# Top-k attention, routed experts and a Fourier mixer on one core: sign and mask of each even tile formed in two parts

## The chip, the cores and the metric

The kernel runs on one core of a Trainium2 chip. The metric is the device time of one execution in microseconds (us); lower is better. The program is written engine by engine: TensorE (PE in the profile, its weight loads PEld), VectorE (DVE), ScalarE (ACT), GpSimd (POOL) and SyncE (SP) each have their own list of instructions, and only semaphores order one list against another.

## The reference, cut to what matters

Three stages follow each other. Only the first is touched by the change.

```python
# attention: batch 4, heads 8, sequence 576, head_dim 64, top_k 32
scores = scale * np.matmul(q, k.transpose(0, 1, 3, 2))
kth = np.partition(scores, -top_k, axis=-1)[..., -top_k:-top_k + 1]
mask = scores >= kth
scores = np.where(mask, scores, -1000000000.0)
attn = softmax(scores)                     # exp, divided by (sum + 1e-9)
out = np.matmul(attn, v)
# then: each token of 2304 is routed to one of 8 experts (512 -> 1024 -> 512, relu), top-1 with a sequential "keep" gate
# then: real part of a 2-D FFT added, layer norm, a 512 -> 2048 -> 512 relu network, added
```

## The kernel before

**Tiles.** The 32 heads are taken in 16 pairs; a pair's 1152 query rows are nine tiles of 128 rows, which makes `NTILE` = 144 tiles of 128 query rows by 576 key columns. Tiles are worked two at a time ("a pair of tiles", t even and t + 1).

**The way of one pair of tiles.** PE forms the scores in two halves of 288 columns (`scores(k, 0)`, `scores(k, 1)`, L467) into two PSUM banks that both halves share, and ACT copies each half into `s_sb` (`evict_scores`, L657), the first halves before the second halves are computed. DVE forms the larger and the smaller of the two halves (`upper`, L797), GpSimd helps with sums (L743, `sums`) and differences (L753, `lowers`), and DVE finds the 32nd largest value with a chain of MAX8 and MATCH_REPLACE8 (`top_op`, L820 and L822), ended by two scans (L826). ACT forms the exponentials `e_sb` (L648), from the 32nd value a bias (L630, L633), and then `sign` (L637): `Sign(score - kth)` over all 576 columns, +1 where the score is kept, -1 where not. GpSimd multiplies `e_sb` by it (L777), so entries that are not kept become negative. PE transposes the tile in five pieces (`turn`, four of 128 columns into bank `ps_t`, L487, and the last 64 columns into a part of `ps_o`, L493), ACT copies them out with Relu, which sets the negative ones to zero (`turned`, L664 and L666), PE multiplies by the values (`values`, L524), and ACT copies the result out (`result`, L676 and L677).

**The order of the work.** Each engine's loop runs `body(t)` for t from -4 to 147, in the order written. PE, at an even t: scores of the first halves of tiles t+4 and t+5; values of tile t-1; some matmuls of other work (from `units_at`, the first experts' blocks, L186, L201 and L213, for t of 84 and more; before that `keep_clock`, filler matmuls that nobody reads, L502); `turn(t)`; scores of the second halves. At an odd t: filler or other work, `turn(t)`, other work, `values(t-1)`. ACT, at an even t: sign of t and t+1, copies of the first halves of the scores, result of t-1, `turned(t)`, copies of the second halves, two exponentials; at an odd t: `turned(t)`, `result(t-1)`. GpSimd, at an even t: two L753, the mask of t; at an odd t: the mask of t+1 of the pair and then two L743. Gathers and scatters of the experts' tokens (L730, L269) stand ahead of the mask in some of these bodies.

**Semaphores around the change.** `s_sign` counts signs, `s_mask` counts masked tiles. `s_mask` releases `turn(k)` on PE (one wait ahead of all five transposes) and, six tiles later, ACT's copy into the same `s_sb` buffer. For the last two tiles DVE forms the mask (L963) instead of ACT and GpSimd.

```python
pe.wait_ge(s_mask, k + 1)                                        # turn(k)
act.activation(s_sb[k % NS][:, :], s_sb[k % NS][:, :], ACT.Sign, ...).then_inc(s_sign, 1)
pool.wait_ge(s_sign, t + 1)
pool.tensor_tensor(e_sb[t % NE][:, :], e_sb[t % NE][:, :], s_sb[t % NS][:, :], ALU.mult).then_inc(s_mask, 1)
```

Of the kernel before, what the change touches and what calls it, by code (L numbers as in the profile page):

```python
# [12 lines left out]
ALU = mybir.AluOpType  # L13
ACT = mybir.ActivationFunctionType
# [3 lines left out]
B, H, S, D = 4, 8, 576, 64  # L18
# [4 lines left out]
P = 128  # L23
# [256 lines left out]
def attention(nc, env, q_h, k_h, v_h, vt_h):  # L280
# [9 lines left out]
    NS, NW, NE, NT_ = 6, 4, 3, 3  # L290
    HALF_TOP = TOPK // 2
    STEPS = 22
    CLOCK = ((6, 3), (9, 8), (5, 3))
    AHEAD = {MIDDLE + 4: 14, MIDDLE + 6: 4, MIDDLE + 8: 4, MIDDLE + 10: 4}
    SCALE = 1.0 / math.sqrt(D)
# [2 lines left out]
    with ExitStack() as ctx:  # L298
# [6 lines left out]
        def sem(name):  # L305
            return ctx.enter_context(nc.semaphore(name))
# [6 lines left out]
        s_sb = [sb(f"s_sb{n}", [P, S]) for n in range(NS)]  # L313
# [5 lines left out]
        nmax, under, ulp = [kept[:, :, 2 * HALF_TOP + 2 + 2 * n:2 * HALF_TOP + 4 + 2 * n] for n in range(3)]  # L319
        e_sb = [sb(f"e_sb{n}", [P, S]) for n in range(NE)]  # L320
# [15 lines left out]
        s_zero, s_mask, s_tr, s_ev, s_pv = sem("s_zero"), sem("s_mask"), sem("s_tr"), sem("s_ev"), sem("s_pv")  # L336
# [113 lines left out]
        def live(k):  # L450
            return 0 <= k < NTILE

        def gates_at(t):
            return t % TPP == TPP - 2 and (t + 2) // TPP < NPAIR

        @block.tensor
        def _(pe):
# [23 lines left out]
                score(k + 1, h).then_inc(s_qk, 1)  # L481

            def turn(k):
                pe.wait_ge(s_mask, k + 1)
                pe.wait_ge(s_ev, 2 * k)
                for c in range(KC):
                    mm = pe.transpose(ps_t[:, c * P:(c + 1) * P], e_sb[k % NE][:, c * P:(c + 1) * P], ident[:, :])  # L487
                mm.then_inc(s_tr, 1)
                if k == 0:
                    pe.wait_ge(s_vg, 2)  # L490
                if k >= 2:
                    pe.wait_ge(s_o, k - 1)
                pe.transpose(ps_o[k % 2][0:S - KC * P, 384:384 + P], e_sb[k % NE][:, KC * P:S], ident[:, :]).then_inc(s_tr, 1)  # L493
# [127 lines left out]
        @block.scalar  # L621
        def _(act):
            act.dma_start(k_sb[0][:, :], k_h[0]).then_inc(s_qk_in[0], 16)

            def sign(k):
                c = k // 2
                if k % 2 == 0:
                    act.wait_ge(s_top, STEPS * c + STEPS)
                    act.wait_ge(s_set, 5)
                    act.activation(ulp[:, c % 2, :], kth[c % 2][:, :, HALF_TOP], ACT.Abs, bias=least[:, :], scale=ULP).then_inc(s_under, 1)  # L630
                    act.wait_ge(s_under, 3 * c + 1)
                    for y in range(2):
                        act.activation(under[:, c % 2, y:y + 1], kth[c % 2][:, y, HALF_TOP:HALF_TOP + 1], ACT.Identity,  # L633
                                       bias=ulp[:, c % 2, y:y + 1], scale=-1.0).then_inc(s_under, 1)
                    act.wait_ge(s_under, 3 * c + 3)
                act.wait_ge(s_exp, k + 1)
                act.activation(s_sb[k % NS][:, :], s_sb[k % NS][:, :], ACT.Sign, bias=under[:, (k // 2) % 2, k % 2:k % 2 + 1],  # L637
                               scale=1.0).then_inc(s_sign, 1)

            def exp(k):  # L640
                c, y = k // 2, k % 2
                if y == 0:
                    act.wait_ge(s_top, STEPS * c + 2)
                    act.activation(nmax[:, c % 2, :], top[c % 2][:, :, 0], ACT.Copy, scale=-SCALE).then_inc(s_nm, 1)
                if k >= NE:
                    act.wait_ge(s_tr, 2 * (k - NE + 1))
                act.wait_ge(s_nm, c + 1)
                act.activation(e_sb[k % NE][:, :], s_sb[k % NS][:, :], ACT.Exp, bias=nmax[:, c % 2, y:y + 1],  # L648
                               scale=SCALE).then_inc(s_exp, 1)

            def evict_scores(k):
                base, h = k - k % 2, k % 2
                for n in (base, base + 1):
                    act.wait_ge(s_qk, 2 * base + 2 * h + n - base + 1)
                    if h == 0 and n >= NS:
                        act.wait_ge(s_mask, n - NS + 1)
                    act.activation(s_sb[n % NS][:, h * SH:(h + 1) * SH], ps_s[n % 2][:, 0:SH], ACT.Copy).then_inc(s_copy, 1)  # L657

            def turned(t):
                pair = eT[t % NT_]  # L660
                act.wait_ge(s_tr, 2 * t + 1)
                if t >= NT_:
                    act.wait_ge(s_pv, t - NT_ + 1)
                act.activation(pair[:, 0:KC, :].rearrange("p c q -> p (c q)"), ps_t[:, :], ACT.Relu).then_inc(s_ev, 1)  # L664
                act.wait_ge(s_tr, 2 * t + 2)
                act.activation(pair[0:S - KC * P, KC, :], ps_o[t % 2][0:S - KC * P, 384:384 + P], ACT.Relu).then_inc(s_ev, 1)  # L666

            def result(k):
                u, rt = k // TPP, ORDER[k % TPP]
                act.wait_ge(s_pv, k + 1)  # L670
                for two in range(2):
                    if (two == 0 and rt > MID) or (two == 1 and rt < MID):
                        continue
                    rows = slice(0, P) if rt != MID else slice(two * HALF, two * HALF + HALF)
                    c0 = two * VW
                    act.activation(gd[rows, rt, u, :], ps_o[k % 2][rows, c0 + D:c0 + VW], ACT.Copy)  # L676
                    op = act.activation(X[rows, rt, u * D:(u + 1) * D], ps_o[k % 2][rows, c0:c0 + D], ACT.Copy)  # L677
                op.then_inc(s_o, 1)

            def body(t):  # L680
                even = t % 2 == 0
                if even and live(t) and t < NTILE - 2:
                    sign(t)
                    sign(t + 1)
                if even and live(t + LQ):
                    evict_scores(t + LQ)
                if even and live(t - 1):
                    result(t - 1)
                if live(t):
                    turned(t)  # L690
                if even and live(t + LQ):
                    evict_scores(t + LQ + 1)
                if even and live(t + LE):
                    exp(t + LE)
                    exp(t + LE + 1)
                if not even and live(t - 1):
                    result(t - 1)
                if gates_at(t):
                    u = (t + 2) // TPP
                    g = v_sb[u % 2][:, :, :].rearrange("p c (w x) -> p c w x", w=2)[:, :, :, D:D + E + 1]  # L700
                    src = ps_o[t % 2][:, GATES:GATES + 2 * (KC + 1) * (E + 1)].rearrange("p (c w e) -> p c w e", w=2, e=E + 1)
                    act.wait_ge(s_vw, u + 1)
                    act.activation(g[:, 0:KC], src[:, 0:KC], ACT.Copy).then_inc(s_vg, 1)
                    act.activation(g[0:S - KC * P, KC], src[0:S - KC * P, KC], ACT.Copy).then_inc(s_vg, 1)
                if t == MIDDLE + 3:
                    act.wait_ge(r["s_sh"], 1)
                    act.activation(r["ex"][:, :, :], r["sh"][:, :, :], ACT.Exp).then_inc(r["s_ex"], 1)
                for kind, j, m in units_at(t):
                    if kind == "x":
                        early_x_out(act, env, j)  # L710
                    elif kind == "h" and m % (NF // 2) == NF // 2 - 1:
                        early_h_out(act, env, j, m // (NF // 2))
                    elif kind == "y" and m == NF - 1:
                        early_y_out(act, env, j)

            run(body)

        @block.gpsimd
        def _(pool):
# [35 lines left out]
            def body(t):  # L755
# [17 lines left out]
                    lowers(t // 2 + 1)  # L773
                if live(t) and t < NTILE - 2:
                    pool.wait_ge(s_exp, t + 1)
                    pool.wait_ge(s_sign, t + 1)
                    pool.tensor_tensor(e_sb[t % NE][:, :], e_sb[t % NE][:, :], s_sb[t % NS][:, :], ALU.mult).then_inc(s_mask, 1)  # L777
                if t % 2 == 1:
                    sums(t // 2 + 2)

# [7 lines left out]
        def _(dve):  # L788
# [170 lines left out]
            dve.wait_ge(s_top, STEPS * (NTILE // 2))  # L959
            for k in range(NTILE - 2, NTILE):  # L960
                dve.wait_ge(s_exp, k + 1)
                dve.wait_ge(s_mask, k)
                dve.scalar_tensor_tensor(e_sb[k % NE][:, :], s_sb[k % NS][:, :], kth[(k // 2) % 2][:, k % 2, HALF_TOP:HALF_TOP + 1],  # L963
                                         e_sb[k % NE][:, :], ALU.is_ge, ALU.mult).then_inc(s_mask, 1)
            early = TPP - LATE
            dve.wait_ge(s_o, LAST + early)
            halves = (slice(0, early // 2), slice(MID + 1, MID + 1 + early // 2))
# [1389 lines left out]
```

## Time and profile before

| what | us |
|---|---|
| median of three runs | 1433.53 |
| lowest and highest of them | 1429.42, 1434.51 |
| the profiled execution, whole time | 1431.98 |
| its span, first to last instruction | 1430.2 |
| attention in it, until the last transpose | about 20 to 696 |
| experts and mixer | about 703 to 1430 |

| engine | busy us | share of the span |
|---|---|---|
| PE | 1370.5 | 96% |
| PEld | 1131.5 | 79% |
| DVE | 980.7 | 69% |
| ACT | 720.1 | 50% |
| POOL | 544.5 | 38% |

Busy time is what an engine's instructions took; the ends of matmuls are modelled, so that a busy PE is not a PE at its peak. The shares are means over stages that have different limits: the stages are told apart in the views by window. "Idle before, releaser" is the time in which an engine did nothing before an instruction, and the instruction of another engine whose semaphore ended it.

### The profile page before, as it was taken

How to read it: one execution, taken by the hardware profiler on the slowest of the kernel's cores; microseconds unless marked ns; L12 is line 12 of the kernel's file. 1: busy time of each engine (PE TensorE's matmuls, PEld its weight loads, DVE VectorE, ACT ScalarE, POOL GpSimd, SP SyncE). 2: the span in 40 equal slices, each digit the busy share in tenths (PEclk: the TensorE clock that was granted, in tenths of full speed). 3: DMA queues.
4: the chain of work that ended last, by engine and by line, in shares of the span. 5: the costliest groups of instructions: out<-in, count | busy, mean ns of one | idle time of the engine just before them, and what ended most of it. 6: DMA issues, size and time to landing. Idle time of an engine off the chain costs nothing. (4 is left out here: it accounts for less than half of the span.)

```text
span 1430.2 us, 25489 instructions
## 1 busy us (share of the span) xinstructions
PE 1370.5 (96%) x8340; PEld 1131.5 (79%) x8340; DVE 980.7 (69%) x3009; ACT 720.1 (50%) x1901; POOL 544.5 (38%) x618
## 2 busy tenths in 40 slices
PE   6999999999999999999999999999999999999998
PEld 4778777777877676677679999967787899999997
DVE  7999999999999899899855545475664323322221
ACT  4877778786657777777534434332222212211110
POOL 3666666666656665675221212121132000000001
PEclk9999999999979999999999999999999999999999
DMA  4110111111172344342447574333211112211111
GB/s 122 35 36 28 36 35 35 36 35 39 64 284 78 123 151 139 114 142 97 160 162 264 184 267 172 138 140 133 97 51 58 46 45 88 89 44 45 55 64 37
DMA packets 76569, 141.93 MB, mean 99 GB/s; under 512 B 27083, under 2 KB 27212, under 8 KB 76442
## 3 DMA queue, kind: packets, MB, share of 16 engines
q1 hardware_dynamic: 57994, 88.43, 18.6%
q10 hardware_dynamic: 11120, 29.66, 5.8%
q0 software_dynamic: 7328, 22.28, 4.4%
q8 instruction: 64, 1.05, 0.3%
q14 instruction: 63, 0.52, 0.1%
HBM read 116.75 MB, written 24.65 MB: 99 GB/s over the span
## 5 line engine op out<-in xcount | busy, mean ns | idle before, releaser
L777 POOL TENSOR_TENSOR e_sb<-e_sb,s_sb 128x576 f32<-128x576 f32 x142 | 198.0, 1412 | 118.3 <-ACT s_sb L637 118.1
L820 DVE MAX8 top<-w_sb 128x8 f32<-128x288 f32 x576 | 233.1, 445 | 0.2
L524 PEld LDWEIGHTS ps_o<-v_sb,eT 128*128 128x128 f32 (+1 forms) x1440 | 187.0, 191 | 44.8 <-issue 30.7
L2068 DVE SCALAR_TENSOR_TENSOR h_lo<-ps_ch,h_hi 128x384 fp32r<-128x384 f32 x96 | 53.4, 556 | 234.7 <-ACT h_hi L1888 234.7
L524 PE MATMUL ps_o<-v_sb,eT 128*128 128x74 f32 (+3 forms) x1440 | 211.1, 284 | 0.3 <-ACT eT L666 0.3
L1888 ACT ACTIVATE h_hi<-ps_ch 128x384 fp32r<-128x384 f32 x96 | 47.2, 491 | 279.8 <-PE ps_ch L1672 279.8
L822 DVE MATCH_REPLACE8 w_sb<-top,w_sb 128x288 f32<-128x288 f32 x432 | 188.0, 443 | 0.0
L743 POOL TENSOR_TENSOR w_sb<-s_sb 128x288 int32<-128x288 int32 x142 | 110.3, 798 | 91.6 <-ACT s_sb L657 91.6
L820 DVE MAX8 ps_l<-w_sb 128x8 f32<-128x288 f32 x288 | 120.8, 454 | 19.1 <-POOL w_sb L753 18.7
L467 PE MATMUL ps_s<-k_sb,q_sb 64*128 64x288 f32 x512 | 115.8, 471 | 17.2 <-DVE w_sb L797 8.0
L1670 PE MATMUL ps_ch<-un_hi,w_hi 128*128 128x384 f32 x384 | 131.1, 342 | 0.6 <-DVE un_lo L2062 0.6
L1672 PE MATMUL ps_ch<-un_hi,w_lo 128*128 128x384 f32 x384 | 129.2, 337 | 0.0
L1671 PE MATMUL ps_ch<-un_lo,w_hi 128*128 128x384 f32 x384 | 128.8, 335 | 0.0
L502 PE MATMUL ps_o<-ident 128*128 128x128 f32 x860 | 123.3, 292 | 0.5 <-ACT rows L677 0.4
L664 ACT ACTIVATE eT<-ps_t 128x512 f32<-128x512 f32 x144 | 84.8, 589 | 76.9 <-PE ps_t L487 76.3
L753 POOL TENSOR_TENSOR w_sb<-w_sb 128x288 int32<-128x288 int32 x142 | 109.8, 794 | 35.5 <-DVE w_sb L797 31.1
L502 PEld LDWEIGHTS ps_o<-ident 128*128 128x128 f32 x860 | 107.1, 198 | 18.4 <-issue 14.1
L1670 PE MATMUL ps_cy<-w_hi,h_hi 128*128 128x512 f32 x288 | 114.4, 397 | 0.0
L1672 PE MATMUL ps_cy<-w_hi,h_lo 128*128 128x512 f32 x288 | 113.4, 394 | 0.0
L1671 PE MATMUL ps_cy<-w_lo,h_hi 128*128 128x512 f32 x288 | 113.1, 393 | 0.0
L487 PE MATMUL ps_t<-ident,e_sb 128*128 128x128 f32 x576 | 91.6, 282 | 22.2 <-POOL e_sb L777 18.3
L657 ACT ACTIVATE s_sb<-ps_s 128x288 f32<-128x288 f32 x288 | 102.6, 401 | 17.5 <-PE ps_s L467 15.1
(333 smaller groups left out, 2664.8 us busy)
## 6 DMA issues: line engine op xcount, KB each, us to landing
w<-in_w SPq DMA_DIRECT2D x18, 2048.0 KB, 13.4
w<-in_w ACTq DMA_DIRECT2D x14, 2048.0 KB, 8.0
stage<-in_w_ch SPq DMA_DIRECT2D x16, 512.0 KB, 5.3
q_sb<-in_q SPq DMA_DIRECT2D x16, 288.0 KB, 2.8
vT<-in_vt SPq DMA_DIRECT2D x16, 288.0 KB, 3.1
x_d<-rows SPq DMA_DIRECT2D x18, 256.0 KB, 2.5
x_d<-u POOLq DMA_DIRECT2D x18, 256.0 KB, 2.8
u<-x_d SPq DMA_DIRECT2D x18, 256.0 KB, 2.8
```

Source lines behind the costliest of these rows:

```text
L467: return pe.matmul(ps_s[k % 2][:, 0:SH], lhsT, k_sb[b][rows, h * SH:(h + 1) * SH], start=True, stop=True)
L502: pe.matmul(ps_o[k % 2][:, 384:384 + P], ident[:, :], ident[:, :], start=True, stop=True)
L524: mm = pe.matmul(ps_o[k % 2][:, lo:hi], eT[k % NT_][0:n, c, :], v_sb[b][0:n, c, lo:hi], start=(c == 0), stop=(c == KC))
L657: act.activation(s_sb[n % NS][:, h * SH:(h + 1) * SH], ps_s[n % 2][:, 0:SH], ACT.Copy).then_inc(s_copy, 1)
L743: pool.tensor_tensor(w[:, SH:S], x[:, 0:SH], x[:, SH:S], ALU.add).then_inc(s_split, 1)
L753: pool.tensor_tensor(w[:, SH:S], w[:, SH:S], w[:, 0:SH], ALU.subtract).then_inc(s_split, 1)
L777: pool.tensor_tensor(e_sb[t % NE][:, :], e_sb[t % NE][:, :], s_sb[t % NS][:, :], ALU.mult).then_inc(s_mask, 1)
L820: dve.max(eight, half).then_inc(s_top, 1)
L822: dve.match_replace(out=half, in_to_replace=eight, in_values=half, imm_value=-BIG).then_inc(s_top, 1)
L1670: pe.matmul(out_, hi1, hi2, start=first, stop=False)
L1671: pe.matmul(out_, hi1, lo2, start=False, stop=False)
L1672: return pe.matmul(out_, lo1, hi2, start=False, stop=last)
```

## The change

The sign and the mask of each even tile become two instructions each, over columns 0 to 255 and 256 to 575; odd tiles keep one. `s_sign` and `s_mask` then count three per pair of tiles: `masked(k)` is the count at which tile k is complete. On PE the wait ahead of `turn(k)` asks, for an even tile, for the first part alone, and a second wait ahead of the third transpose asks for the second part. The mask of the last two tiles, by DVE, counts two and one so that the numbers fit. No buffer, no order of instructions and no amount of data changes.

```diff
+    FIRST = 2 * P
...
+        def parts(k):
+            return [slice(0, FIRST), slice(FIRST, S)] if k % 2 == 0 else [slice(0, S)]
+
+        def masked(k):
+            return 3 * (k // 2) + 2 + k % 2
...
             def turn(k):
-                pe.wait_ge(s_mask, k + 1)
+                pe.wait_ge(s_mask, masked(k) - 1 + k % 2)
                 pe.wait_ge(s_ev, 2 * k)
                 for c in range(KC):
+                    if k % 2 == 0 and c * P == FIRST:
+                        pe.wait_ge(s_mask, masked(k))
                     mm = pe.transpose(ps_t[:, c * P:(c + 1) * P], e_sb[k % NE][:, c * P:(c + 1) * P], ident[:, :])
...
                 act.wait_ge(s_exp, k + 1)
-                act.activation(s_sb[k % NS][:, :], s_sb[k % NS][:, :], ACT.Sign, bias=under[:, (k // 2) % 2, k % 2:k % 2 + 1],
-                               scale=1.0).then_inc(s_sign, 1)
+                for cols in parts(k):
+                    act.activation(s_sb[k % NS][:, cols], s_sb[k % NS][:, cols], ACT.Sign,
+                                   bias=under[:, (k // 2) % 2, k % 2:k % 2 + 1], scale=1.0).then_inc(s_sign, 1)
...
                     if h == 0 and n >= NS:
-                        act.wait_ge(s_mask, n - NS + 1)
+                        act.wait_ge(s_mask, masked(n - NS))
...
                     pool.wait_ge(s_exp, t + 1)
-                    pool.wait_ge(s_sign, t + 1)
-                    pool.tensor_tensor(e_sb[t % NE][:, :], e_sb[t % NE][:, :], s_sb[t % NS][:, :], ALU.mult).then_inc(s_mask, 1)
+                    for n, cols in enumerate(parts(t)):
+                        pool.wait_ge(s_sign, masked(t) - len(parts(t)) + n + 1)
+                        pool.tensor_tensor(e_sb[t % NE][:, cols], e_sb[t % NE][:, cols], s_sb[t % NS][:, cols],
+                                           ALU.mult).then_inc(s_mask, 1)
...
                 dve.wait_ge(s_exp, k + 1)
-                dve.wait_ge(s_mask, k)
+                dve.wait_ge(s_mask, masked(k - 1))
                 dve.scalar_tensor_tensor(e_sb[k % NE][:, :], s_sb[k % NS][:, :], kth[(k // 2) % 2][:, k % 2, HALF_TOP:HALF_TOP + 1],
-                                         e_sb[k % NE][:, :], ALU.is_ge, ALU.mult).then_inc(s_mask, 1)
+                                         e_sb[k % NE][:, :], ALU.is_ge, ALU.mult).then_inc(s_mask, 2 - k % 2)
```

## Rows read from the trace of the kernel before

**Rows 1.** By window: start:end, length, then each engine's busy us (x instructions), PEclk, DMA.

```profile
20.00:330.00 310.00, 294.05 (x2056) 239.12 (x2055) 308.80 (x1135) 245.67 (x736) 208.49 (x213) 0.99 0.11 32
330.00:430.00 100.00, 94.53 (x657) 79.97 (x655) 96.38 (x349) 60.81 (x179) 61.82 (x64) 0.91 0.39 138
430.00:540.00 110.00, 105.10 (x674) 78.41 (x674) 98.78 (x355) 83.01 (x244) 69.67 (x71) 1.00 0.35 114
540.00:690.00 150.00, 144.10 (x880) 104.06 (x880) 136.67 (x493) 115.96 (x337) 95.96 (x97) 1.00 0.36 124
```

**Rows 2.** Waits: PE in 430 to 690, then DVE in 20 to 700.

```profile
PE ps_t L487 <- POOL e_sb L777: 9.6, 13, 1.3
...
DVE ps_l L820 <- POOL w_sb L753: 18.7, 46, 1.7
DVE w_sb L797 <- ACT s_sb L657: 9.0, 12, 1.4
```

**Rows 3.** Timeline of one pair of tiles, 540.86 to 546: start, length, engine, line.

```profile
540.86 1.44 ACT L637 ACTIVATE s_sb<-s_sb,kept 128x576 f32<-128x576 f32 x2
...
541.78 2.77 POOL L777 TENSOR_TENSOR e_sb<-e_sb,s_sb 128x576 f32<-128x576 f32 x2 [3.71 <-ACT s_sb L637]
...
542.21 0.69 ACT L657 ACTIVATE s_sb<-ps_s 128x288 f32<-128x288 f32 x2
...
543.24 0.66 PE L487 MATMUL ps_t<-ident,e_sb 128*128 128x128 f32 x4 [1.29 <-POOL e_sb L777]
...
543.93 0.60 ACT L664 ACTIVATE eT<-ps_t 128x512 f32<-128x512 f32 x1 [0.85 <-PE ps_t L487]
...
543.93 0.76 PE L467 MATMUL ps_s<-k_sb,q_sb 64*128 64x288 f32 x4
...
545.16 0.82 DVE L797 TENSOR_TENSOR w_sb<-s_sb,ps_s 128x288 f32<-128x288 f32 x2 [1.02 <-ACT s_sb L657]
...
545.58 0.60 PE L487 MATMUL ps_t<-ident,e_sb 128*128 128x128 f32 x4
```

**Rows 4.** ScalarE's groups, shapes apart, whole span.

```profile
L657 ACT ACTIVATE s_sb<-ps_s 128x288 f32<-128x288 f32 x288 | 102.6, 401 | 17.5 <-PE ps_s L467 15.1
L637 ACT ACTIVATE s_sb<-s_sb,kept 128x576 f32<-128x576 f32 x142 | 102.4, 768 | 2.3
L664 ACT ACTIVATE eT<-ps_t 128x512 f32<-128x512 f32 x144 | 84.8, 589 | 76.9 <-PE ps_t L487 76.3 <-issue 0.3
...
L633 ACT ACTIVATE kept<-kept 128x1 f32<-128x1 f32 x142 | 34.1, 287 | 2.3
```

**Rows 5.** GpSimd's groups, shapes apart, whole span.

```profile
L777 POOL TENSOR_TENSOR e_sb<-e_sb,s_sb 128x576 f32<-128x576 f32 x142 | 198.0, 1412 | 118.3 <-ACT s_sb L637 118.1
L743 POOL TENSOR_TENSOR w_sb<-s_sb 128x288 int32<-128x288 int32 x142 | 110.3, 798 | 91.6 <-ACT s_sb L657 91.6
...
L2195 POOL TENSOR_TENSOR xb<-xb,hi 128x255 f32<-128x255 f32 x8 | 6.6, 827 | 0.0
```

**Rows 6.** PE's timeline: four of the seven long waits ahead of an even tile's transposes.

```profile
421.98 1.11 PE L487 MATMUL ps_t<-ident,e_sb 128*128 128x128 f32 x4 [1.74 <-POOL e_sb L777]
...
512.25 0.66 PE L487 MATMUL ps_t<-ident,e_sb 128*128 128x128 f32 x4 [0.44 <-POOL e_sb L777]
...
600.76 0.66 PE L487 MATMUL ps_t<-ident,e_sb 128*128 128x128 f32 x4 [0.58 <-POOL e_sb L777]
...
658.17 0.66 PE L487 MATMUL ps_t<-ident,e_sb 128*128 128x128 f32 x4 [1.33 <-POOL e_sb L777]
```

**Rows 7.** A pair of tiles with a scatter of GpSimd between its two masks.

```profile
484.22 0.66 PE L487 MATMUL ps_t<-ident,e_sb 128*128 128x128 f32 x4 [0.74 <-POOL e_sb L777]
...
484.32 1.03 POOL L269 DMA_INDIRECT y_d<-stage,early_sidx  x1 [0.16 <-issue]
...
486.85 0.66 PE L487 MATMUL ps_t<-ident,e_sb 128*128 128x128 f32 x4 [1.18 <-POOL e_sb L777]
```

**Rows 8.** By window: a stretch with a lower granted clock (the column after POOL's).

```profile
420.00:428.00 8.00, 6.26 (x27) 4.94 (x27) 7.84 (x30) 5.35 (x15) 5.23 (x6) 0.59 0.42 149
```

## The prediction

> **What bounds the kernel now.** I read the busy times by window first, because the page's shares are means over stages [rows 1]. In 20 to 330 us DVE is busy 308.8 of 310 us: the chain of MAX8 and MATCH_REPLACE8 is the bound, 35 pairs of tiles at about 8.7 us each, and PE's 294 us contain filler matmuls. In 330 to 430 DVE also carries the routing (96.4 of 100 us). From 430 to 690 the picture turns: PE is busy 105.1 of 110 and 144.1 of 150 us, 249.2 of 260, with real work (the first experts' blocks) where filler stood before, and DVE 235.5 of 260. So the second stage, some 27 pairs of tiles, is bound by PE or by a round through PE; the first by DVE.
>
> Then the waits [rows 2]. Of PE's 10.8 idle us in 430 to 690, 9.6 lie ahead of the transposes L487, ended by GpSimd's mask L777. DVE has waits of its own: 18.7 us for L753 and 9.0 us for ScalarE's copy L657, nearly all of them after 400. Who causes them shows in the timeline of one pair [rows 3]: both signs start at 540.86, the mask of the even tile at 541.78, its transposes at 543.24 after PE idled 1.29 us; the second halves of the scores stand behind the transposes on PE (543.93), ScalarE copies them, and only then can DVE go on at 545.16, after 1.02 us idle. So mask, transposes, scores, copy, DVE is one chain, and its first links are what the change cuts. In the first stage the same chain has slack: it ends before DVE asks.
>
> **The change part by part.**
>
> *Sign, on ScalarE.* One instruction of 576 columns takes 768 ns [rows 4]. Two copies of 288 and 512 columns give the slope, (589 - 401) / 224 = 0.84 ns a column, and 768 - 576 x 0.84 = 284 ns is left as the fixed part; L633, of one column, with 287 ns says the same. So 256 columns take 0.50 us, 320 columns 0.55 us. Two signs back to back take 1.44 us, so they start 0.67 apart and overlap by 0.10: an added instruction costs 0.28 - 0.10 = 0.19 us of ScalarE. The first part is done 0.27 earlier than the whole was, the second at 0.40 + 0.55 = 0.95 after the sign's start, the odd tile's sign 0.19 later.
>
> *Mask, on GpSimd.* 576 columns take 1.41 us, and nothing before runs this instruction on 256 or 320 columns. Two rows bound it [rows 5]: 288 columns of an integer add, 0.80 us, leave a fixed part of 0.80 x 2 - 1.41 = 0.18 us and 0.73 and 0.87 us for the parts; 255 float columns of the mixer, 0.83 us, give (1.41 - 0.83) / 321 = 1.8 ns a column, a fixed part of 0.37, and 0.83 and 0.94 us. Two masks start 1.36 apart, an overlap of 0.05. I take the middle.
> The Trainium skill (GPSIMD Engine Reference, 3.1 Elementwise) gives a two-input operation some 2.6 cycles an element at 1.2 GHz; from that the 576 columns need 1.25 us and 0.16 is fixed. By that the lower bound of the mask's parts holds, and the sum below would be 2.7 rather than 2.3 us; this trace, which has no such float instruction of half the length beside it, can't decide.
>
> *When the transposes can start.* Count from the start of the sign [rows 3]. Before: mask from 0.92 (0.15 after the sign's end) to 2.33, first transpose at 2.38, third 0.27 later at 2.65 (four take 0.66, each 0.28, so they start 0.13 apart). After: first mask from 0.50 + 0.15 = 0.65 to 1.38 or 1.48; the second follows at once, since its sign (0.95) is long there, and ends at 2.20 or 2.37; the third transpose starts at 2.25 or 2.42. The first two can go from about 1.45 on, as soon as PE is free. So where PE waited for the mask, the four transposes end 0.23 to 0.40 us earlier, whatever the length of the wait: a wait of 1.3 us doesn't vanish, it moves mostly to a place between the second and the third transpose. I take 0.33. A wait shorter than that vanishes. The odd tile's mask ends between 0.12 earlier and 0.10 later, at nothing: its transposes come 2.3 us after the even ones (545.58 after 543.24) and do not wait in an ordinary pair.
>
> *The added wait on PE.* Behind it stand transposes three to five, the second halves of the scores, all the later work. It costs a restart: four transposes take 0.66 us after a wait and 0.60 without [rows 3], so 0.06 us, inside my 0.33. Where PE comes late and both parts are there I cost it at nothing, since the wait is met before PE reads it; the other bound is the same 0.06 us.
 It speaks against the change; with the restart in every even tile the sum would fall to near nothing, which is the second rival.
>
> *ScalarE's 0.19 us.* It lies ahead of the copies of the first halves (542.21 to 542.90, needed by scores at 543.93, 0.8 us to spare now, 0.4 to 0.5 after) and of `turned`, which waits 0.85 us for the transposes [rows 3]. With transposes 0.33 earlier and ScalarE 0.19 later, 0.33 of the 0.85 is left. Hidden, but if the slack were gone it would cost 0.19 us a pair. GpSimd's added 0.13 to 0.32 us lies in its waits for the sign, 118 us in all [rows 5].
>
> *The sum.* In the first stage nothing: DVE has no idle time to give back, and PE's shorter wait there becomes a longer wait for DVE. From 400 on there are seven waits of 0.4 us or more ahead of an even tile's transposes in an ordinary pair: 1.74 at 421.98, 1.26 at 472.99, 0.44 at 512.25, 1.29 at 543.24, 0.44 at 561.41, 0.58 at 600.76 and 1.33 at 658.17 [rows 3, 6]. 7 x 0.33 = 2.3 us. Waits of about 0.1 in three more pairs add 0.3. Not counted are pairs in which a gather or scatter of GpSimd stands between the masks: there the odd tile waits again (1.18 us at 486.85 [rows 7]) and swallows what the even one won. That holds for four pairs; and a wait of 0.44 at 609.33, after which DVE is busy without a break up to its next scan, 0 or 0.3. The sum is 2.6 us, with bounds of 7 x 0.23 = 1.6 and 7 x 0.40 + 0.3 + 0.4 = 3.5 us. What is late next is the same wait, for the second part of the mask, and behind it DVE's chain, which has 24 us idle in 430 to 690 and so lets the gain through.
> Against its own time the profiled execution would come to 1431.98 - 2.6 = 1429.4 us. It lay 1.55 us below the median of the three runs, so the median goes to 1433.53 - 2.6 = **1430.9 us**. The three runs span 5 us, so this is a change that is hardly to be told from none; 0.5% (7.2 us) is about what a measurement of this kernel can tell.
>
> **The rivals.**
>
> *All of PE's waits go.* If the gain per pair were not capped by the second part, PE's 9.6 us of [rows 2] and the 1.74 at 421.98 would go: 1433.5 - 11.3 = 1422.2 us. For it: PE is the busiest engine there, and DVE's waits hang on the same chain. Against: the third transpose can't start before 2.25 us after the sign, and the waits of 1.3 us, which hold half of the sum, end at 2.38. Chance 0.06.
>
> *Nothing is left of it.* The restart of 0.06 us in each of some 36 even tiles after 330 costs 2.2 us, or the won time is swallowed by another wait further on: 1433.5 us. For it: in most pairs there is no wait to shorten, and PE pays each of its instructions there. The rule on weight loads that is named above would do this. Against: a met wait should cost no restart. Chance 0.22.
>
> *Slower: ScalarE's extra instruction lies on the round.* In 430 to 690 a round goes sign, mask, transposes, values, result, next bias, next sign, with ScalarE's list in fixed order. If the 0.85 us ahead of L664 [rows 3] is not slack in the pairs that PE leads, 0.19 us a pair is paid in all 36 pairs after 330, 6.8 us, and with GpSimd's 0.18 (lower price) on the odd mask 13.3 us: 1440.4 to 1446.8 us. It decides from the point at which ScalarE reaches `turned` later than the transposes end, which needs 0.5 us more than now. Against: the wait of 0.85 stands in nearly every even tile after 430. Chance 0.07.
>
> *The clock.* At 420 to 428 the granted clock was 0.59, so for the larger part the lower level, 1.2 GHz [rows 8], just after filler and the 1.74 us wait, and the odd tile's transposes came 4.4 us after the even ones instead of 2.3: about 2 us. The change moves idle time of PE about; one such stretch fewer gives 1428.9, one more 1432.9. Only four more would reach 0.5%. Chance that this decides the sign: 0.1, within "same" but for 0.01.
>
> **How the numbers follow.** Forecast 0.55, all waits go 0.06, nothing left 0.22, ScalarE on the round 0.07, clock 0.10. Faster by over 0.5%: 0.06 and a little of the forecast's tail, 0.07. Slower by over 0.5%: 0.07 and 0.01 of the clock, 0.08. Within 0.5%: 0.85. The range takes in the forecast's bounds, a clock stretch either way, the second rival and half of the runs' spread of 5 us: 1430.9 - 0.9 - 2 - 2.5 = 1425.5 below, 1433.5 + 2.5 = 1436 above.
>
> **What would show it.** Right: in the changed kernel's timeline an even tile's transposes come as two and two (start of the third 2.25 to 2.42 us after the sign); PE's waits at L487 in 430 to 690 fall from 9.6 by 2 to 3 us, the rest standing ahead of the third transpose; ScalarE's wait for L487 shrinks from 0.85 to about 0.35; DVE in 20 to 330 stays at 99 to 100% with the same length of pair; the last transposes of attention come 2 to 3 us earlier than 696. Wrong: the parts of the mask together longer than 1.9 us (GpSimd's fixed cost over 0.4), a longer period in the first stage, a wait of DVE at L797 there, or a different number of stretches at the lower clock.

## The result, and the profile after

| kernel | median us | lowest, highest | profiled execution, span |
|---|---|---|---|
| before, 10 runs beside it | 1433.40 | 1429.42, 1439.51 | 1430.2 |
| after, 10 runs | 1439.76 | 1435.50, 1441.75 | 1439.5 |

The ratio is 1.0041, 95% interval 1.0023 to 1.0058: slower, by 6 us, where 2.6 us less was forecast; 1439.76 lies above the range. The ratios leave out two executions of e3 that lay over 1.5% above its fastest; the medians leave out none. Here are the windows of after that answer to [rows 1]:

```profile
20.00:330.00 310.00, 296.45 (x2015) 242.35 (x2013) 302.54 (x1109) 247.00 (x755) 208.39 (x243) 0.96 0.11 32
330.00:430.00 100.00, 94.00 (x665) 79.70 (x663) 97.46 (x349) 63.64 (x194) 64.32 (x74) 0.93 0.39 137
430.00:540.00 110.00, 107.18 (x656) 80.44 (x655) 98.94 (x358) 83.69 (x250) 69.62 (x81) 0.96 0.32 110
540.00:690.00 150.00, 147.11 (x898) 107.91 (x897) 136.53 (x492) 117.86 (x352) 98.96 (x115) 0.98 0.38 128
```

The first line holds the surprise. DVE, which had been busy 308.8 of the 310 us, is busy 302.5, and the granted clock of TensorE is 0.96 where it was 0.99. PE is *busier*, 296.5 for 294.1 us, with fewer matmuls done (2015 for 2056): it works slower. In windows of 10 us one sees where:

```profile
190.00:200.00 10.00, 9.12 (x45) 7.87 (x44) 10.00 (x39) 5.52 (x16) 5.87 (x7) 0.69 0.01 2
230.00:240.00 10.00, 10.00 (x45) 8.08 (x46) 8.56 (x33) 5.12 (x16) 4.63 (x6) 0.66 0.01 2
310.00:320.00 10.00, 9.12 (x43) 7.69 (x41) 9.99 (x38) 5.34 (x17) 5.49 (x7) 0.66 0.00 0
```

The same windows of before show 1.00 and 65 to 69 matmuls. After has six such stretches at the lower level (1.2 GHz) between 190 and 345 us, five of them up to 330, 3.4 or 6.8 us long each, where before had one of 3.4 us in the whole first stage, at 118 us. (A "fall" is the start of such a stretch below, and its time is that at which the granted clock drops.) And this is what PE waited for, in 20 to 330 and then in 430 to 690 us (compare [rows 2]):

```profile
PE ps_s L474 <- DVE w_sb L809: 10.9, 15, 1.0
...
PE ps_t L496 <- POOL e_sb L788: 4.9, 11, 1.4
```

In 20 to 330 us before waited 6.8 us for the mask (18 waits, 0.4 at most) and 5.7 us for DVE (14, 0.5 at most). After has no wait for the mask there of a length that the view lists, and 10.9 us for DVE, up to 1.0 at a time. PE's timeline around the first fall, before first and then after:

```profile
189.70 0.66 PE L487 MATMUL ps_t<-ident,e_sb 128*128 128x128 f32 x4 [0.36 <-POOL e_sb L777]
...
194.32 0.72 PE L467 MATMUL ps_s<-k_sb,q_mid 128*128 128x288 f32 x2 [0.54 <-DVE w_sb L797]
```

```profile
187.41 0.84 PE L496 MATMUL ps_t<-ident,e_sb 128*128 128x128 f32 x4
...
192.56 0.72 PE L474 MATMUL ps_s<-k_sb,q_mid 128*128 128x288 f32 x2 [0.88 <-DVE w_sb L809]
193.21 0.77 PE L474 MATMUL ps_s<-k_sb,q_sb 64*128 64x288 f32 x2
193.91 2.62 PE L533 MATMUL ps_o<-v_sb,eT 128*128 128x74 f32 x10
```

The two idle times 0.36 and 0.54 have become one of 0.88. The clock falls at 193.8 us, and the ten matmuls L533 from 193.91 on take 2.62 us, where ten such take 1.48 at the full level.

Lining up the even tiles' transposes of the two profiled executions shows where most of the 9.3 us between their spans come from. After is ahead by 2.3 us at tile 38 (0.9 to 1.5 of them from the start of the execution, 1 from before's own fall at 118 us). It is behind by 0.7 at tile 40, 2.8 at tile 48, 4.1 at tile 52, 7.3 at tile 66 and 8.4 at tile 70: one step at each fall, of 0.6 to 3 us, 10.7 us in all. From there to tile 134 it *gains* 2.3 us, though a fall at 494 us costs 2.5 of its own. A fall at 661 us takes some of that back, and at tile 142 it is 7.1 us behind. The other 2.2 us arise behind the attention, where the change alters nothing: the stretch at the lower clock that begins at 713 us is 6.8 us long, and before's at 708 is 3.4. They were not traced further.

### The profile page after: what moved, and what is told of

It is laid out like the page before. It is cut to its first block and busy times, and to the rows that moved or that the text cites. A ratio compares the mean times of both kernels' runs of the same rounds, so it can differ in the third digit from the quotient of the medians.

```text
span 1439.5 us, 25632 instructions
## 1 busy us (share of the span) xinstructions
PE 1384.9 (96%) x8340; PEld 1145.6 (80%) x8340; DVE 982.1 (68%) x3009; ACT 732.9 (51%) x1972; POOL 554.4 (39%) x689
## 5 line engine op out<-in xcount | busy, mean ns | idle before, releaser
L788 POOL TENSOR_TENSOR e_sb<-e_sb,s_sb 128x256 f32<-128x256 f32 (+2 forms) x213 | 208.1, 1003 | 99.9 <-ACT s_sb L647 99.7
L533 PEld LDWEIGHTS ps_o<-v_sb,eT 128*128 128x128 f32 (+1 forms) x1440 | 190.2, 194 | 45.1 <-issue 29.2
L533 PE MATMUL ps_o<-v_sb,eT 128*128 128x74 f32 (+3 forms) x1440 | 214.7, 288 | 0.3 <-ACT eT L676 0.3
L511 PE MATMUL ps_o<-ident 128*128 128x128 f32 x860 | 129.6, 302 | 0.5 <-ACT rows L687 0.4
L511 PEld LDWEIGHTS ps_o<-ident 128*128 128x128 f32 x860 | 112.8, 207 | 18.6 <-issue 14.1
L647 ACT ACTIVATE s_sb<-s_sb,kept 128x256 f32<-128x256 f32 (+2 forms) x213 | 115.6, 605 | 2.3
```

The lines of the kernel that those rows point to most:

```text
L511: pe.matmul(ps_o[k % 2][:, 384:384 + P], ident[:, :], ident[:, :], start=True, stop=True)
L533: mm = pe.matmul(ps_o[k % 2][:, lo:hi], eT[k % NT_][0:n, c, :], v_sb[b][0:n, c, lo:hi], start=(c == 0), stop=(c == KC))
L647: act.activation(s_sb[k % NS][:, cols], s_sb[k % NS][:, cols], ACT.Sign, bias=under[:, (k // 2) % 2, k % 2:k % 2 + 1], scale=1.0).then_inc ...
L788: pool.tensor_tensor(e_sb[t % NE][:, cols], e_sb[t % NE][:, cols], s_sb[t % NS][:, cols], ALU.mult).then_inc(s_mask, 1)
```

## The experiments

Two theories stood against each other. **Idle:** gathered idle time of PE in the first stage is followed by stretches at the lower clock, in which PE falls behind DVE. **Instructions:** the added signs, masks and waits cost the time. Before's own median in these sessions was 1432.75 (e1 to e4), 1433.39 (e5 to e8) and 1434.85 us (e9, e10), and the ratios are against it.

| run | median us | ratio to before, 95% interval |
|---|---|---|
| e1 joined release | 1434.62 | 1.0005, 0.9989 to 1.0021 |
| e2 two parts late only | 1431.67 | 0.9987, 0.9971 to 1.0004 |
| e3 before, idle gathered | 1447.37 | 1.0088, 1.0061 to 1.0116 |
| e4 after, filled | 1428.97 | 0.9968, 0.9954 to 0.9982 |
| e5 two parts early only | 1438.35 | 1.0044, 1.0027 to 1.0061 |
| e6 after, filled apart | 1429.26 | 0.9964, 0.9950 to 0.9977 |
| e7 before, filled apart | 1430.20 | 0.9977, 0.9966 to 0.9988 |
| e8 after, half filled | 1431.89 | 0.9990, 0.9978 to 1.0001 |
| e9 joined release, filled apart | 1430.11 | 0.9973, 0.9954 to 0.9992 |
| e10 e6 with more filler | 1427.93 | 0.9965, 0.9946 to 0.9984 |

**e1_join: the parts without the early release.**

```diff
-                pe.wait_ge(s_mask, masked(k) - 1 + k % 2)
+                pe.wait_ge(s_mask, masked(k))
...
-                    if k % 2 == 0 and c * P == FIRST:
-                        pe.wait_ge(s_mask, masked(k))
```

> The changed kernel, but PE waits for both parts of an even tile's mask ahead of its first transpose; signs and masks are still formed in two parts. Theory idle (PE's idle time of the first stage, two waits of 0.37 and 0.54 us a pair in the kernel before, was gathered by the early release into one of 0.88 us, and stretches at the lower clock follow it): the two waits are apart again, at most 2 low stretches in 20 to 330 us, 1430 to 1434 us. Theory instructions (the added instructions of ScalarE and GpSimd or their semaphores cost the time): 1438 us or more, with DVE waiting in 20 to 330 at full clock.

Measured: 1434.62 us, ratio 1.0005: all added instructions of ScalarE and GpSimd are there, and the loss is gone. PE's waits in 20 to 330 us are spread again, in 38 waits of at most 0.7 us, and DVE is full:

```profile
20.00:330.00 310.00, 293.04 (x2068) 238.25 (x2069) 309.95 (x1143) 254.21 (x777) 214.57 (x251) 1.00 0.11 32
...
PE ps_s L474 <- DVE w_sb L807: 9.1, 19, 0.7
PE ps_t L494 <- POOL e_sb L786: 4.7, 19, 0.3
```

So it is the release, not the instructions, that makes the loss. The median is 0.6 us above what was expected of idle. The profiled execution has no fall in 20 to 330 us, though eleven of PE's waits for DVE there are of 0.62 to 0.67 us, longer than before's 0.54. Over all its executions e1's mean granted clock, 0.984, still lies below before's 0.988; its profile has falls from 357 us on, the first behind a wait of 1.08 us.

**e2_late and e5_early: one stage at a time.** The parts are formed for even tiles from 86 on (e2) or below 72 (e5); all counts follow from `parts`.

```diff
+        def split(k):
+            return k >= EARLY0 + 2          # e5_early: k < MIDDLE
+
         def parts(k):
-            return [slice(0, FIRST), slice(FIRST, S)] if k % 2 == 0 else [slice(0, S)]
+            return [slice(0, FIRST), slice(FIRST, S)] if k % 2 == 0 and split(k) else [slice(0, S)]
```

> The changed kernel with two parts only for even tiles from 86 on, one part before that. Theory idle: nothing changes in the first stage, the second gains what was predicted for it: 1430 to 1432.5 us, 1 or 2 low stretches up to 330 us. Theory instructions: 29 of 71 added pairs of instructions remain, so a loss of about 2.5 us, 1435 to 1437 us.

> The changed kernel with two parts only for even tiles below 72, one part from 72 on: the other half of the run with two parts from 86 on. Theory idle: the whole loss sits here, so the changed kernel's 6 us over before plus the 1 to 2.5 us that the late half gained: 1439 to 1443 us, 3 or more low stretches in 20 to 330 us. Theory instructions: half of the added instructions, so half of the loss: 1436 us.

Measured: e2 1431.67 us (ratio 0.9987, interval just over 1), e5 1438.35 (1.0044). e2 has no fall up to 330 us, where 1 or 2 were expected. The whole loss sits in the first stage, the second stage by itself comes out at or a little under before. e5 fell short of the 1439 expected of idle by 0.7 us, and is further from the 1436 of the other theory. Its profile has falls at 72, 154, 171 and 270 us. The first three stand behind waits of 0.87 to 0.93 us, the fourth behind one of 0.53:

```profile
60.00:80.00 20.00, 19.10 (x106) 15.14 (x105) 18.88 (x70) 13.99 (x42) 11.94 (x14) 0.81 0.07 16
150.00:160.00 10.00, 9.12 (x49) 7.54 (x49) 10.00 (x39) 6.30 (x21) 5.18 (x6) 0.83 0.00 1
```

**e3_gathered: the loss without the change.** The kernel before, with its nine filler matmuls a pair placed eight and one instead of six and three.

```diff
-    CLOCK = ((6, 3), (9, 8), (5, 3))
+    CLOCK = ((8, 1), (9, 8), (5, 3))
```

> The kernel before, no parts at all, with the filler of the first stage placed otherwise: 8 and 1 matmuls ahead of the even and odd tile's transposes, where 6 and 3 were, so as many in all. The even tile's wait for the mask goes, and the idle time gathers ahead of the scores, 0.9 us. Theory idle: at least 4 low stretches in 20 to 330 us and 1436 to 1442 us. Theory instructions: no added instruction, no loss: 1432 to 1435 us.

Measured: 1447.37 us (1446.8 without the two executions that its ratio leaves out), ratio 1.0088, so the loss comes without any part and is larger than expected. The profile has four falls in 20 to 330 us, at 91, 118, 197 and 217 us, as many as were expected at the least. PE's idle time is gathered in one wait, and three of the four falls stand behind such a wait:

```profile
195.53 0.72 PE L467 MATMUL ps_s<-k_sb,q_mid 128*128 128x288 f32 x2 [0.99 <-DVE w_sb L797]
196.19 0.86 PE L467 MATMUL ps_s<-k_sb,q_sb 64*128 64x288 f32 x2
196.98 2.62 PE L524 MATMUL ps_o<-v_sb,eT 128*128 128x74 f32 x10
199.53 3.78 PE L502 MATMUL ps_o<-ident 128*128 128x128 f32 x16
```

The 16 matmuls are the eight filler ones: at the lower level they hold the transposes up for 3.8 us, where after's twelve took 2.93. On the line-up of the tiles this fall costs 3.4 us, after's at 194 us 3.0. That may be why e3 loses more than its clock explains: its mean granted clock of 0.977 would make a loss of about 10 us by the slope given further down, and its median is 14.6 us over before's. It was not tried apart, so e3 shows that gathering brings the falls, and not that they are the whole of its loss.

**e4_filled, e6_filled_apart, e8_half_filled: filling the gathered wait.** Filler goes ahead of the scores of those pairs in which after waited 0.5 to 0.9 us; in e4 into the bank `ps_o` (behind a wait for ScalarE's copies), in e6 and e8 into a bank that is free then.

```diff
+    FILL = {12: 3, 16: 3, 2: 2, 4: 3}            # e8: {12: 1, 16: 1, 2: 1, 4: 1}
...
+                if 8 < t < MIDDLE and t % 18 in FILL:
+                    keep_clock_apart(FILL[t % 18])    # e4: keep_clock(t, FILL[t % 18])
                 if t in AHEAD:
```

> The changed kernel with 2 or 3 filler matmuls more in the first stage, ahead of the scores of those pairs of tiles in which PE idled 0.5 to 0.9 us there. Theory idle: at most 1 low stretch in 20 to 330 us, DVE there at 99 to 100%, 1428 to 1432 us. Theory instructions: 1438 to 1441 us, as the changed kernel, since PE has more to do and not less.

> The changed kernel with filler ahead of the scores of the same pairs as in the filled run, the same number, but into a bank that nobody else uses then, so that the filler waits for nothing (in the filled run it waited 8.4 us for ScalarE's copies in 20 to 330 us). Theory idle: no low stretch in 20 to 330 us and DVE busy there at 99% or more: 1426.5 to 1429.5 us. If the filled run's gain came from another order of the work and not from PE's activity, this one differs from it by its absent waits alone; either way over 1433 us would speak against idle.

> The changed kernel with one filler matmul (0.27 us) in each of those pairs, so that the wait of 0.88 us becomes about 0.6. Theory idle: fewer low stretches in 20 to 330 us than in the changed kernel (7 of all 12), more than with full filler, and a time between: 1430 to 1437 us. Theory instructions: 1439 us.

Measured: 1428.97, 1429.26 and 1431.89 us, ratios 0.9968, 0.9964 and 0.9990. More work on PE makes the changed kernel 8 to 11 us faster than without it. In 20 to 330 us, e4, e6 and e8:

```profile
20.00:330.00 310.00, 299.25 (x2107) 245.58 (x2108) 305.47 (x1123) 249.52 (x763) 210.67 (x245) 1.00 0.11 32
```

```profile
20.00:330.00 310.00, 306.19 (x2150) 247.95 (x2151) 310.00 (x1143) 254.54 (x776) 214.89 (x250) 1.00 0.11 32
```

```profile
20.00:330.00 310.00, 300.79 (x2099) 242.41 (x2100) 310.00 (x1143) 254.85 (x777) 215.20 (x251) 1.00 0.11 32
```

None has a fall there. DVE is busy all 310 us in e6 and e8. In e4 it was not (305.5, against the 99% expected). PE waited 8.4 us in 14 waits for ScalarE's copies before its filler, but that is the smaller part of it: 3.3 of DVE's 4.5 idle us lie in 30 to 50 us, because in this execution TensorE came to the full clock later. Ten matmuls of 74 columns at 30.5 us still took 2.62 us, in e6 those at 28.9 us took 1.48. One filler matmul in place of two or three, which leaves PE waits of at most 0.5 us, already kept the clock in the profiled execution; the expectation of e8 puts seven of after's falls into 20 to 330 us, the trace has five. Filler of the same amount at another place of the pair was not tried, so that it has to stand in the wait itself is argued, not shown.

**e7_before_filled and e9_joined_filled: what the filler is worth by itself.** The kernel before, and e1, each with the filler of e6.

> The kernel before, no parts, with the same filler as in the filled-apart run. Theory idle: its two short waits a pair rarely bring a low stretch, so the filler gains little: 1430 to 1433 us, and two parts are worth 2 to 3 us once the clock is kept (this run less the filled-apart one). Theory instructions: the same gain from filler as in the changed kernel, 8 us or more: 1425 us.

> The filled-apart kernel, but PE waits for both parts ahead of the first transpose. With the clock kept in the first stage, this prices the added instructions of ScalarE and GpSimd without the early release. If they cost nothing and only the release gains: as the kernel before with the same filler, 1430 to 1431.5 us. If they cost 0.1 us or more in each of the 36 pairs after 330 us: 1433 us or more.

Measured: 1430.20 and 1430.11 us, ratios 0.9977 and 0.9973, both times as expected. Filler gains 0.23% in the kernel before and about 0.8% in the changed one (from 1.0041 to 0.9964). With the clock kept, neither the added instructions (e9 against e7) nor the early release (e6 against e9, 0.9964 to 0.9973) move the time beyond the intervals. The 2 to 3 us that two parts were to be worth (e7 less e6) are 1.9 us by the ratios, and not resolved.

**e10_more_filler: a fall of the second stage.**

```diff
+    MORE = {99: 4, 109: 2}
...
+                    if t in MORE:
+                        keep_clock(t, MORE[t])
                     turn(t)
```

> The filled-apart kernel with 4 filler matmuls ahead of the transposes of tile 99 (1.1 us, PE waits 1.4 us there for the mask behind a scatter) and 2 ahead of tile 109 (0.7 us wait). Theory idle: the stretch at the lower clock that begins in these 1.4 us (484 us) goes, and 1 to 2.5 us with it: 1426.5 to 1428 us. If low stretches of the second stage have another cause, the stretch at 484 us stays and the time is 1429 us; the one at 651 us, ahead of which PE has no wait, stays in either case.

Measured: 1427.93 us, ratio 0.9965. The profiles of e6 and e10 around tile 99, in this order:

```profile
481.59 0.44 PE L497 MATMUL ps_t<-ident,e_sb 128*128 128x128 f32 x2 [0.39 <-POOL e_sb L791]
...
484.22 0.90 PE L497 MATMUL ps_t<-ident,e_sb 128*128 128x128 f32 x4 [1.40 <-POOL e_sb L791]
...
485.13 1.91 PE L201 MATMUL ps_a<-stage,w 128*128 128x128 f32 x8
```

```profile
480.20 1.16 PE L513 MATMUL ps_o<-ident 128*128 128x128 f32 x8
481.68 0.65 PE L498 MATMUL ps_t<-ident,e_sb 128*128 128x128 f32 x4 [0.32 <-POOL e_sb L794]
...
482.28 1.06 PE L201 MATMUL ps_a<-stage,w 128*128 128x128 f32 x8
```

The fall in the wait is gone: eight matmuls L201 take 1.06 us again instead of 1.91. No gain over e6 shows: 0.9965 against 0.9964 by the ratios, where 1 to 2.5 us were expected. The fall at 651 us was expected to stay and is absent in this one profiled execution, as in those of before and e7; the nine others have it, at 650 to 664 us. In none of them did PE wait in the 10 us before it. What starts it stays open; what PE did ahead of it stands in the last section.

## Why the prediction was wrong

**The step that failed** is the first sentence of the sum: "In the first stage nothing: DVE has no idle time to give back, and PE's shorter wait there becomes a longer wait for DVE." The half sentence was right almost to the hundredth, 0.36 and 0.54 became 0.88 us. The "nothing" was not: the first stage cost 10.7 us on the line-up of the tiles. A wait of PE in a stage that DVE bounds costs nothing by itself, but gathered it was followed by the lower clock behind six of the eleven waits of 0.88 to 0.98 us between 60 and 345 us, and each such stretch made PE the late one and cost 0.6 to 3 us. e3 shows the falls without the change, e1 and e6 take the loss away with the parts in place. The prediction had named the signs of this among those of being wrong, a longer period in the first stage and another number of stretches at the lower clock.

**The clock rival** named the right thing. Its price was about right, 2 us for a stretch (the steps at tiles 40 to 70 average 10.7 / 6 = 1.8 us). Its count was wrong: "only four more would reach 0.5%", with 0.01 of chance for the slower side. I had counted the falls of before and asked how often the lot would fall differently. The change shortened one kind of wait in all 36 even tiles of the stage and lengthened another, so the count was free to grow in a whole stage. It grew from one to six in the profiled executions. The two rows of waits, 6.8 us for the mask in 18 and 5.7 for DVE in 14, stand in before's trace, and I didn't add them pair by pair.

**The times of the parts** were right, at the lower bound. The changed kernel's groups are

```profile
L788 POOL TENSOR_TENSOR e_sb<-e_sb,s_sb 128x320 f32<-128x320 f32 x71 | 61.4, 865 | 0.0
L788 POOL TENSOR_TENSOR e_sb<-e_sb,s_sb 128x256 f32<-128x256 f32 x71 | 52.2, 735 | 99.7 <-ACT s_sb L647 99.7
...
L647 ACT ACTIVATE s_sb<-s_sb,kept 128x320 f32<-128x320 f32 x71 | 38.8, 547 | 0.0
...
L647 ACT ACTIVATE s_sb<-s_sb,kept 128x256 f32<-128x256 f32 x71 | 36.1, 508 | 2.3
```

so 0.74 and 0.87 us for the mask (0.73 and 0.87 from the integer row, 0.83 and 0.94 from the mixer's), and 0.51 and 0.55 for the sign (0.50 and 0.55). The middle that I took for the mask was wrong by 0.1 us. The rows give (1.41 - 0.87) / 256 = 2.1 ns a column and 0.74 + 0.87 - 1.41 = 0.20 us as the fixed part. The Trainium skill's 2.6 cycles an element (GPSIMD Engine Reference, 3.1 Elementwise) make an estimate of 2.2 ns and 0.16 us, with which this trace agrees within 0.04 us.

**Two and two.** An even tile that waits looks as predicted:

```profile
548.71 1.63 ACT L647 ACTIVATE s_sb<-s_sb,kept 128x256 f32<-128x256 f32 x3
...
549.36 2.92 POOL L788 TENSOR_TENSOR e_sb<-e_sb,s_sb 128x256 f32<-128x256 f32 x3 [3.27 <-ACT s_sb L647]
...
550.14 0.44 PE L496 MATMUL ps_t<-ident,e_sb 128*128 128x128 f32 x2 [0.32 <-POOL e_sb L788]
...
550.96 0.44 PE L496 MATMUL ps_t<-ident,e_sb 128*128 128x128 f32 x2 [0.39 <-POOL e_sb L788]
...
551.44 0.60 ACT L674 ACTIVATE eT<-ps_t 128x512 f32<-128x512 f32 x1 [0.33 <-PE ps_t L496]
```

The third transpose starts 550.96 - 548.71 = 2.25 us after the sign (2.25 to 2.42 predicted), and ScalarE's wait of 0.85 is now 0.33 (about 0.35 predicted). The rival that put ScalarE's extra 0.19 us on the round had the right sign of the result and not its cause: e9 keeps the added instructions and loses nothing. The rival of the restart between the transposes is answered by the trace as well: in 16 of after's 26 even tiles from 86 to 141 outside the stretches at the lower clock, the third transpose starts 0.11 us after the second, as in before, so a wait that is met costs nothing there. Where it is not met, at 550.96 above, the weight load of the third transpose starts together with its matmul. The Trainium skill (TensorE: Matmul & The Clock Gate, Step-by-step: what each phase is for) has PE pull weight loads ahead of running matmuls. Here none is pulled ahead, and a loss from it shows in no ratio.

**The second stage** gained what was added up for it, or more. e7 and e10 have no fall between 430 and 690 us; from tile 86 to tile 142 the kernel with parts gains 3.8 us on the one without, where 2.6 were forecast, with bounds of 1.6 and 3.5 (e10's filler ahead of tiles 99 and 109 is in that). e9, whose transposes wait for both parts, gains 1.1 us on e7 from tile 86 to tile 134, so that not all of it is the early release. These are single executions, and the ratios of whole runs do not resolve the gain. PE's waits there fell from 9.6 to 4.9 us, 4.7 where 2 to 3 were expected, but that is not a larger gain: the first two transposes now run in what was waiting time, 1.29 us became 0.32 and 0.39. In the changed kernel falls at 494 and 661 us took much of it back.

**Do the sizes meet?** In 33 runs of the kernel before (the session of e1 to e4), time falls with the run's mean granted clock by 0.97 us for each 0.001 (correlation -0.94). The mean clock of after's ten runs was 0.9766 against 0.9878 in those 33, which by that slope is 10.8 us; 6.4 were lost. The 4 to 5 us between them are about the second stage's gain; this is an estimate from the slope, not a measurement. e6, at 0.9872, runs at before's clock and is 4 us faster.

## What to carry to other kernels

When a change shortens a wait of TensorE in a stage that another engine bounds, follow the idle time to its new place, pair by pair: the sum stays, but two short waits may become one long one, and the granted clock answers to where it lies. Read the window table of the granted clock beside every such change, over several executions, and treat filler that keeps the clock as tuned to the waits of its kernel; if they move, it has to move too. Here the change together with two or three filler matmuls in the gathered wait (e6, e10) is 0.35% faster than before, the change alone 0.4% slower. Filler without the change (e7) already gives 0.23%, and the difference between the two is not resolved.

## What the runs showed of the hardware

**Falls behind waits.** In the first stage, with PE otherwise busy, 12 of the 31 waits of 0.86 us or more from 30 to 345 us in the profiled executions of after, e5 and e3 (6 of 11, 3 of 9, 3 of 11) were followed, within 3 us, by 3.4 to 10.2 us at 1.2 GHz, and the others were not. Pairs with waits of 0.37 and 0.54 us apart had one fall in 300 us (before). Eleven waits of 0.62 to 0.67 us had none (e1), waits of at most 0.5 us none (e8), each in one profiled execution; a wait of 0.53 us in e5 had one behind it.

**Falls without a wait.** A fall also came with no wait of PE ahead of it. At 651.7 us in e6 one begins, and the window 652 to 656 us shows

```profile
652.00:656.00 4.00, 4.00 (x18) 3.38 (x19) 3.56 (x14) 3.08 (x10) 2.91 (x3) 0.50 0.83 278
```

so idle time, as the trace records it, is not the only thing that goes before one. Up to 700 us the twelve profiled executions have 21 falls ahead of which PE waited for nothing in 8 us, the unchanged kernel's at 394 us among them. In all 21, matmuls of only 18 or 21 columns stood closely ahead, the last of them at most 2.5 us. In e6 they are these, ahead of its falls at 392 and 651.7 us:

```profile
389.54 2.19 PE L567 MATMUL ps_a<-early_what,early_at_pos 128*128 128x21 f32 x18
...
649.02 1.29 PE L549 MATMUL ps_o<-wg_sb,vT 128*128 128x18 f32 x10
```

About nine in ten groups of such matmuls were followed by no fall, and no run changed them, so that they have a part in it is not shown.
